# First stage of agent attention with an MLP: a ones column behind each value tile, 98-column key scores, and another order of the stage's work

## The chip, the cores and the metric

One core of a Trainium2 chip runs the kernel. The metric is device time in microseconds (us); the kernel before took 935.32 us, median of 3 runs.

## The reference

Two batches of 12480 queries, keys and values (128 channels) meet 49 agents. Then an MLP of 128 to 2048 to 128 channels with a PReLU runs over the 24960 rows.

```python
def sm(a, b):
    s = scale * (a @ b.transpose(0, 2, 1))
    s = s - s.max(-1, keepdims=True)
    e = np.exp(s)
    return e / (e.sum(-1, keepdims=True) + 1e-09)
a2k = sm(agents, k)
agent_v = a2k @ v
q2a = sm(q, agents)
attn = q2a @ agent_v
h = x @ w_in                       # x is attn, batch after batch
g = np.maximum(h, 0.0) + alpha * np.minimum(h, 0.0)
return g @ w_out
```

## The kernel before, in words

The main stage handles 52 chunks of 480 queries. `agent_v` is mixed into `w_in` ahead of it ("mix": `M_a`, `M_r`, and `L_a`, `L_b` for the linear part), so that a chunk is one product of its softmax `PT` with `M`, a ReLU split into `r_hi` and `r_lo`, and the second layer. The mixing needs `agent_v` of the batch. For batch 1 it is computed inside the first chunks of the main stage; for batch 0 it is computed in a stage of its own, the first stage, which takes the first 80 us or so. The change is there.

The first stage of before, each engine in the order in which its code is written (there is no scheduler; semaphores join them):

1. Keys. Tile 0 is a tail of two times 96 keys, then 12 pieces of 8 tiles of 128 keys. SyncE's queue (SP) loads a piece into a ring of 4 slots of `kv_s`; TensorE scores it against `agents` (L407), which holds the 98 agent columns of both batches and 30 columns of zeros, ScalarE saves the scores into `S` (L831), VectorE takes the maximum (L978). Between the pieces stand a maximum over the ReLU weights (L1141, L455, L459) and the scale and split of `w_out` (`weight_scale`, `weights_high` L860, `weights_low` L1087).
2. The maximum over all keys goes over TensorE to every partition (L446, L450) and into `k_shift`; GpSimd subtracts it from each piece (L381), ScalarE takes the exponential (L835).
3. TensorE turns the weights of the MLP (`turn_weights`, L431, 4 groups), scores the first two query chunks (L520), multiplies `w_in` by the linear `w_out` (`linear_weights`, L438), and multiplies each exponentiated piece with its values (`first_values`, L483: `S` is the stationary operand with 49 columns, the value tile streams through with 128 columns, even and odd tiles on two halves of the array). VectorE sums each piece (L1003) for the softmax denominators; `key_sums`, `key_sum` and `denominators` (L493) bring them to every partition, L1179 takes the reciprocal.
4. Handing over: `turn_values` (L489), `value_sums` (L497), `mix` (L501), `mix_rest`, `mix_linear`, the first `tiles` (L539) of the main stage, and then its first second layer (L556).

Queries of a chunk pass: scores on TensorE, `query_shift`, `query_exp`, `query_sum`, `query_norm`, then `query_hi` (ScalarE), `query_again` (GpSimd) and `query_lo` (VectorE, L1115) into `stack`. Once all three are there, SP's `turn(n, half)` issues four transposing DMAs `PT<-stack` (L275), waits until they have landed, and issues three copies `PR<-PT` (L279). SP is one queue in order: in the main stage it loads `q_s` for chunk n + 3 (L297) only after `turn(n + 1)`, and TensorE scores that chunk in the fourth second layer of chunk n:

```python
pe.wait_ge(in_q[1 - half], 16 * i + 32 + 16 * half)
...
second_layer(3, half, scores)
```

In chunk 0 this is `q_s[1]` with chunk 3, issued after `turn(1, 1)`, which waits for `query_lo(1)`.

Of the kernel before, what the change touches and what calls it, by code (L numbers as in the profile page):

```python
# [20 lines left out]
PIECE = 8 * KT  # L21
TAIL = (N - FULL * PIECE) // 2
# [19 lines left out]
def build(nc, kT, kTail, vP, vS, vTail, qT, agT, w_inT, w_out, alpha_col, out):  # L42
    ctx = ExitStack()
    with ctx:
# [9 lines left out]
        agents = sb("agents", [C, 128])  # L54
# [25 lines left out]
        kv_s = sb("kv_s", [128, 2 * RING, PIECE])  # L80
        k_tail = sb("k_tail", [C, B, 2 * TAIL])
        v_tail = sb("v_tail", [TAIL, B, 2 * C])
# [9 lines left out]
        av_rows = sb("av_rows", [128, C])  # L92
# [46 lines left out]
        def slot(p):  # L139
# [14 lines left out]
        consts, stack_zero, pool_step, dve_step = sem("consts"), sem("stack_zero"), sem("pool_step"), sem("dve_step")  # L154
# [10 lines left out]
        b_col, b_row, b_diag, b_top, b_shift, b_sum, b_den, b_dened, b_rows, b_turned, b_abs, b_vsum, b_vmax, b_av, b_avl = (  # L165
            sem(x) for x in ("b_col", "b_row", "b_diag", "b_top", "b_shift", "b_sum", "b_den", "b_dened", "b_rows",
# [55 lines left out]
        def value_tile(m, t):  # L222
            return kv_s[:, value_slot(m), t * C:(t + 1) * C]
# [4 lines left out]
        def _(sp):  # L228
            def load_keys(m):
                s = (m - 1) % RING  # L230
                if m > RING:

                    sp.wait_ge(k_scored, m - RING + 1)
                sp.dma_start(kv_s[:, s, :], kT[0, m - 1]).then_inc(in_k[s], 16)
# [15 lines left out]
            sp.dma_start(w_inT_s[:, :, :], w_inT).then_inc(in_wT, 16)  # L250
            for n in range(2):
                sp.dma_start(q_s[:, n, :], qT[n]).then_inc(in_q[n], 16)
            sp.dma_start(v_tail[:, 0, :], vTail[0]).then_inc(in_vt[0], 16)
            for m in range(1, FULL + 1):
                load_values(m)
# [25 lines left out]
            turn(0, 0)  # L281
# [3 lines left out]
            sp.dma_start(kv_s[:, 2, :], kT[1, 0]).then_inc(in_k[2], 16)  # L285
            for h in range(2):
                sp.dma_start(kv_s[:, h, :], kT[1, EARLY + h - 1]).then_inc(in_k[h], 16)
            sp.dma_start(v_tail[:, 1, :], vTail[1]).then_inc(in_vt[1], 16)
            turn(1, 1)

            def body(i, b, kind):
                for half in range(2):
# [30 lines left out]
        def _(pool):  # L323
            pool.memset(agents[:, B * A:128], 0.0).then_inc(consts, 1)
# [4 lines left out]
            pool.memset(rec_sel[:, :], 0.0).then_inc(consts, 1)  # L329
# [31 lines left out]
            pool.wait_ge(consts, 7)  # L361
# [42 lines left out]
        def _(pe):  # L404

            def wide_score(src, rows, bank, t):
                return pe.matmul(ps[0:rows, bank, t * 128:(t + 1) * 128], src, agents[:, :], start=True, stop=True)  # L407
# [61 lines left out]
            def first_values(m):  # L469
# [3 lines left out]
                else:  # L473
                    pe.wait_ge(in_v[(m - 1) % (2 * RING)], 16 * ((m - 1) // (2 * RING) + 1))
                pe.wait_ge(k_exped, m + 1)
                for t in range(count):
                    if m == 0:
                        rhs, rows = v_tail[:, 0, t * C:(t + 1) * C], TAIL
                    else:
                        rhs, rows = value_tile(m, t), KT  # L480

                    side = t % 2 * 64
                    mm = pe.matmul(ps[side:side + A, OUT, 0:C], S[0:rows, 0, at + t, :], rhs, start=(m == 0),  # L483
# [819 lines left out]
```

## Time and profile before

| | |
|---|---|
| median of 3 runs (lowest, highest) | 935.32 us (934.98, 936.42) |
| the profiled execution, its time and its span | 934.78 us, 933.1 us |
| TensorE (PE) busy | 98% of the span |
| VectorE, ScalarE, GpSimd busy | 68%, 55%, 12% |
| granted TensorE clock, mean | 0.992 |

The span runs from the first to the last instruction; the difference to the time lies around it. PE busy counts overlapping matmuls once, so 98% says that TensorE is seldom empty, not that it works at its peak. A float32 matmul stands in the profile as two instructions. The granted clock is 1.00 for 2.4 GHz and 0.50 for 1.2 GHz.

### The profile page before, as it was taken

To read this page: it belongs to the slowest core of one execution; us is meant where nothing else is said; L and a number is where in the kernel's file an instruction comes from. 1 tells how busy PE (TensorE), PEld (TensorE's weight loads), DVE (VectorE), ACT (ScalarE), POOL (GpSimd) and SP (SyncE) were. 2 spreads that over 40 slices of the span, in tenths; PEclk is the share of its full clock that TensorE was granted. 3 is DMA by queue.
4 is the path that set the end of the run, shared out by engine and by line. 5 is a ranking of instruction groups with operands and counts; after the bars stand their busy time and mean duration, and the time that the engine had idled before them with its cause. 6 is when DMAs were issued, how large, how long until landed. Compare 5 with 4: busy or idle time off the path is not lost.

```text
span 933.1 us, 16065 instructions
## 1 busy us (share of the span) xinstructions
PE 913.1 (98%) x5642; PEld 489.6 (52%) x5642; DVE 636.1 (68%) x927; ACT 514.6 (55%) x694; POOL 108.7 (12%) x140
## 2 busy tenths in 40 slices
PE   7899999999999999999999999999999999999998
PEld 6775555555545655654544444444444444444443
DVE  4567676676677777776776667676767676767664
ACT  2235555555556555555556555555555555555654
POOL 6310100100101001001001010101010101010101
PEclk9799999999999999999999999999999999999999
DMA  8751232222222322211111111111111111111110
GB/s 294 280 175 57 61 100 59 74 82 60 84 75 72 118 71 72 87 34 53 39 38 57 34 50 43 50 42 49 44 43 50 40 52 41 52 39 53 40 33 22
DMA packets 63206, 65.76 MB, mean 70 GB/s; under 512 B 38528, under 2 KB 57280, under 8 KB 62912
## 3 DMA queue, kind: packets, MB, share of 16 engines
q1 hardware_dynamic: 62880, 65.19, 22.9%
q8 instruction: 24, 0.39, 0.2%
q14 instruction: 14, 0.11, 0.0%
q10 hardware_dynamic: 288, 0.06, 0.0%
HBM read 40.49 MB, written 12.78 MB: 57 GB/s over the span
## 4 chain that ended last, share of the span: by engine, by line
PE 92%; DVE 2%; DMA 2%; issue 2%; SPq 1%; ACT 1%; POOLq 0%; POOL 0%
PE ps L556 54%; PE ps L539 17%; PE ps L546 7%; PE ps L520 3%; PE ps L566 2%; PE ps L718 2%; PE ps L407 2%; PE ps L712 1%; PE ps L483 1%; DMA kv_s<-kT 1%; PE ps L431 1%; PE ps L501 1%; DMA q_s<-qT 1%; SPq L275 0%; PE ps L438 0%
## 5 line engine op out<-in xcount | busy, mean ns | idle before, releaser
L1120 DVE SCALAR_TENSOR_TENSOR r_lo<-ps,r_hi 128x960 f16<-128x960 f32 x416 | 466.6, 1153 | 249.4 <-ACT r_hi L879 247.0
L879 ACT ACTIVATE r_hi<-ps 128x960 f16<-128x960 f32 x416 | 386.2, 967 | 175.4 <-PE ps L546 175.3
L556 PE MATMUL ps<-r_hi,w_hi 128*128 128x480 f16 x832 | 252.1, 369 | 1.9 <-DMA q_s<-qT 1.1
L556 PE MATMUL ps<-r_hi,w_lo 128*128 128x480 f16 x832 | 248.0, 366 | 0.0
L556 PE MATMUL ps<-r_lo,w_hi 128*128 128x480 f16 x832 | 240.7, 366 | 0.0
L539 PE MATMUL ps<-PT,M_a 128*128 128x480 f16 x832 | 203.3, 366 | 0.3 <-DVE r_lo L1120 0.2
L392 POOL TENSOR_TENSOR y<-y_relu,y_lin 128x480 f32<-128x480 f32 x52 | 62.4, 1200 | 616.6 <-ACT y_relu L958 444.3
L556 PEld LDWEIGHTS ps<-r_hi,w_lo 128*128 128x128 f16 x832 | 91.3, 110 | 68.8
L539 PEld LDWEIGHTS ps<-PT,M_a 128*128 128x128 f16 x832 | 81.1, 99 | 86.6 <-DVE r_lo L1120 2.6
L556 PEld LDWEIGHTS ps<-r_lo,w_hi 128*128 128x128 f16 x832 | 85.4, 106 | 71.2
L556 PEld LDWEIGHTS ps<-r_hi,w_hi 128*128 128x128 f16 x832 | 73.0, 106 | 85.3 <-issue 44.6
L941 ACT ACTIVATE y_lin<-ps,lin_unscale 128x480 f32<-128x480 f32 x52 | 34.4, 661 | 85.8 <-PE ps L566 85.8
L546 PE MATMUL ps<-PR,M_r 32*128 32x480 f16 x624 | 78.7, 372 | 0.0
L546 PE MATMUL ps<-PT,M_r 32*128 32x480 f16 x208 | 77.3, 371 | 0.0
L520 PEld LDWEIGHTS ps<-agents,q_s 128*120 128x120 f32 x416 | 70.3, 186 | 7.7 <-issue 0.4
L520 PE MATMUL ps<-agents,q_s 128*120 128x49 f32 x416 | 64.8, 242 | 0.0
L546 PEld LDWEIGHTS ps<-PT,M_r 32*128 32x128 f16 x208 | 18.8, 90 | 82.6 <-issue 82.2
L958 ACT ACTIVATE y_relu<-ps,out_unscale 128x480 f32<-128x480 f32 x52 | 34.4, 661 | 35.7 <-PE ps L556 35.7
L871 ACT ACTIVATE stack<-q_p 120x196 f16<-120x196 f32 x52 | 19.4, 373 | 62.1 <-DVE q_p L1111 62.1
L373 POOL TENSOR_TENSOR stack<-stack,ones 120x120 f16<-120x120 f16 x52 | 20.9, 402 | 181.1 <-ACT stack L871 181.1
L718 PEld LDWEIGHTS ps<-S,kv_s 128*128 128x128 f32 x192 | 33.1, 190 | 1.2
L712 PEld LDWEIGHTS ps<-agents,kv_s 128*128 128x128 f32 x176 | 30.9, 191 | 1.1
(143 smaller groups left out, 530.0 us busy)
## 6 DMA issues: line engine op xcount, KB each, us to landing
q_s<-qT SPq DMA_DIRECT2D x52, 240.0 KB, 2.7
out<-y SPq DMA_DIRECT2D x52, 240.0 KB, 2.0
kv_s<-kT SPq DMA_DIRECT2D x24, 512.0 KB, 4.1
kv_s<-vP SPq DMA_DIRECT2D x12, 512.0 KB, 7.6
kv_s<-vS SPq DMA_DIRECT2D x8, 768.0 KB, 4.3
PR<-PT SPq DMA_DIRECT2D x156, 32.0 KB, 1.9
PT<-stack SPq DMA_TRANSPOSE x208, 2.4
w_lin<-w_out SPq DMA_DIRECT2D x1, 1024.0 KB, 7.8
```

Source lines behind the costliest of these rows:

```text
L373: pool.tensor_tensor(stack[0:T, :, 2 * A:128], stack[0:T, :, REST:A], ones[0:T, 0:4 * SPARE].rearrange("p (t a) -> p t a", a=SPARE), ALU.m ...
L392: pool.tensor_tensor(y[:, half, :], y_relu[:, half, :], y_lin[:, half, :], ALU.add).then_inc(y_ready, 1)
L520: return pe.matmul(ps[0:T, SMALL, t * A:(t + 1) * A], q_s[:, half, t * T:(t + 1) * T], agents[:, b * A:(b + 1) * A], start=True, stop=True)
L539: pe.matmul(by_tile(ps[:, 2 * slot(p) + u, 0:CHUNK]), M_a[:, b, f:f + 128], tokens(PT, half), start=True, stop=False)
L546: mm = pe.matmul(by_tile(ps[:, 2 * slot(2 * q + u // 2) + u % 2, 0:CHUNK]), M_r[32 * u:32 * u + 32, b, q * 128:(q + 1) * 128], tokens(src[ ...
L556: mm = pe.matmul(ps[:, OUT, 0:CHUNK], w[:, 2 * p + u, :], r[:, s, u, :], start=(p == 0 and u == 0 and k == 0), stop=(p == PAIRS - 1 and u ...
L712: mm = pe.matmul(ps[:, SMALL, t * A:(t + 1) * A], kv_s[:, half, t * KT:(t + 1) * KT], agents[:, A:2 * A], start=True, stop=True)
L718: mm = pe.matmul(ps[:, SMALL, 0:A], second_s[:, at:at + C], S[:, 1, SECOND * n + (t + 2 - SECOND * FIRST_VALUES), :], start=(t == 0), stop ...
L879: act.activation(r_hi[:, p % RING, :, :], ps[:, at:at + 2, 0:CHUNK], ACT.Relu).then_inc(hi_ready, 1)
L941: act.activation(y_lin[:, half, :], ps[:, 2 * LIN_SLOT, 0:CHUNK], ACT.Copy, scale=lin_unscale[:, b, :]).then_inc(lin_saved, 1)
L958: act.activation(y_relu[:, half, :], ps[:, OUT, 0:CHUNK], ACT.Copy, scale=out_unscale[:, b, :]).then_inc(relu_saved, 1)
L1120: dve.scalar_tensor_tensor(out=r_lo[:, p % RING, :, :], in0=ps[:, at:at + 2, 0:CHUNK], scalar=0.0, in1=r_hi[:, p % RING, :, :], op0=ALU.ma ...
```

## The change

- Value tiles stand 129 columns apart in `kv_s` (`VC = C + 1`), each with a column of ones behind it, set by VectorE (`ones_of`). `first_values` streams 129 columns, so that column 128 of the product is the sum of the exponentials, the softmax denominator. A load of values is now written as 8 runs of 128 floats in each partition in place of one of 1024.
- For batch 0 `piece_sum`, `key_sums`, `key_sum` and `denominators` go. In their place: both halves of the denominator column scale the selection matrix (`den_sel`, one instruction each on VectorE and ScalarE), `denominators_spread` multiplies with ones (160 columns), VectorE adds EPS and takes the reciprocal over 128x160. Batch 1 keeps its sums.
- `agents` has 98 columns, without the zeros; wide scores stream 98 columns.
- TensorE: all of `turn_weights` stands around the exchange of the maxima, ahead of the values; `relu_max_row` moves from piece 7 to piece 10, `relu_max_everywhere` from piece 8 to after the turning; `linear_weights` moves ahead; the scores of chunk 2 (L520) move from behind the first `rest_of_quad` to between `value_sums` and the second half of the key tiles of batch 1.
- VectorE and ScalarE: `weight_scale`, `weights_high` and `weights_low` leave the key pieces and go behind the maxima; the shift of chunk 2 stands ahead of the first `mixed_low`, `query_lo(1)` behind the second, and the two key maxima of batch 1 behind `relu_lo(1, 1)`.
- SP: `w_lin` is loaded after the third key piece instead of the second, `w_inT` after the tenth, `q_s` of chunk 1 behind the first values, `turn(0, 0)` behind the first key load of batch 1.

```diff
-        agents = sb("agents", [C, 128])
+        agents = sb("agents", [C, B * A])
-        kv_s = sb("kv_s", [128, 2 * RING, PIECE])
+        kv_s = sb("kv_s", [128, 2 * RING, 8 * VC])
...
-                sp.dma_start(kv_s[:, value_slot(m), :], vP[m - 1]).then_inc(in_v[(m - 1) % (2 * RING)], 16)
+                sp.dma_start(values_in(m)[:, :, 0:C], vP[m - 1].rearrange("p (t c) -> p t c", c=C)).then_inc(in_v[(m - 1) % (2 * RING)], 16)
...
-                if m == 2:
+                if m == 3:
                     sp.dma_start(w_lin[:, :, :], w_out).then_inc(in_wo, 16)
+                if m == FULL - 2:
+                    sp.dma_start(w_inT_s[:, :, :], w_inT).then_inc(in_wT, 16)
...
-            turn(0, 0)
             sp.dma_start(k_tail[:, 1, :], kTail[1]).then_inc(in_kt[1], 16)
             sp.wait_ge(v_used, 2 * RING + 1)
-            sp.dma_start(kv_s[:, 2, :], kT[1, 0]).then_inc(in_k[2], 16)
+            sp.dma_start(kv_s[:, 2, 0:PIECE], kT[1, 0]).then_inc(in_k[2], 16)
+            turn(0, 0)
...
+            def denominators_spread():
+                pe.wait_ge(b_spread, 2)
+                pe.matmul(ps[:, K_BANK, 0:SEL], ones[:, :], den_sel[:, :], start=True, stop=True).then_inc(b_den, 1)
...
             act.wait_ge(v_used, FULL + 1)
-            act.activation(av_rows[64:64 + A, :], ps[64:64 + A, OUT, 0:C], ACT.Copy).then_inc(b_rows, 1)
+            act.activation(av_rows[64:64 + A, :], ps[64:64 + A, OUT, 0:VC], ACT.Copy).then_inc(b_rows, 1)
+            act.wait_ge(b_rows, 2)
+            act.activation(den_sel[64:64 + A, :], sel[64:64 + A, :], ACT.Copy,
+                           scale=av_rows[64:64 + A, C:VC]).then_inc(b_spread, 1)
...
+            dve.tensor_copy(av_rows[0:A, :], ps[0:A, OUT, 0:VC]).then_inc(b_rows, 1)
+            dve.wait_ge(b_rows, 2)
+            dve.tensor_scalar(den_sel[0:A, :], sel[0:A, :], av_rows[0:A, C:VC], None, ALU.mult).then_inc(b_spread, 1)
+            dve.wait_ge(b_den, 1)
+            dve.tensor_scalar(rec_sel[:, :], ps[:, K_BANK, 0:SEL], EPS, None, ALU.add).then_inc(b_dened, 1)
             dve.wait_ge(b_dened, 1)
-            then(dve.reciprocal(rec[:, :], den[:, :]))
+            then(dve.reciprocal(rec_sel[:, :], rec_sel[:, :]))
```

Where the order moves, first on TensorE (PE), from the first key piece to the first value tiles. Before:

```order
L407 MATMUL ps<-agents,kv_s 128x128 x56
L455 MATMUL ps<-ident,w_col 1x128
L407 MATMUL ps<-agents,kv_s 128x128 x8
L459 MATMUL ps<-relu_top,ones 128x1
L407 MATMUL ps<-agents,kv_s 128x128 x32
L446 MATMUL ps<-ident,k_col 49x128
L450 MATMUL ps<-k_diag,ones 128x49
L431 MATMUL ps<-turn_sign,w_inT_s 128x128 x4
L520 MATMUL ps<-agents,q_s 120x49 x4
L483 MATMUL ps<-v_tail,S 49x128 x2
```

TensorE of the change, the same place (L418 are the key scores, L442 the turned weights, L457 and L461 the exchange of the maxima, L449 the linear weights):

```order
L418 MATMUL ps<-agents,kv_s 128x98 x80
L466 MATMUL ps<-ident,w_col 1x128
L418 MATMUL ps<-agents,kv_s 128x98 x16
L442 MATMUL ps<-turn_sign,w_inT_s 128x128 x8
L457 MATMUL ps<-ident,k_col 49x128
L442 MATMUL ps<-turn_sign,w_inT_s 128x128 x4
L461 MATMUL ps<-k_diag,ones 128x49
L442 MATMUL ps<-turn_sign,w_inT_s 128x128 x4
L470 MATMUL ps<-relu_top,ones 128x1
L538 MATMUL ps<-agents,q_s 120x49 x4
L449 MATMUL ps<-w_lin,w_inT_s 128x128 x6
L496 MATMUL ps<-v_tail,S 49x129 x2
```

The two small matmuls leave the middle of the key pieces, and the weights' turning now fills the places of the two exchanges. Then VectorE (DVE) at the handing over, from the rest's low half to the second ReLU residue. Before (L1115 is `query_lo(1)`, L978 the two key maxima of batch 1, L1097 and L1099 the shift of chunk 2):

```order
L1077 TENSOR_TENSOR M_r<-ps,M_rh 128x512
L1115 TENSOR_TENSOR stack<-q_p,stack 120x4x49
L1081 SCALAR_TENSOR_TENSOR L_a<-L_a,gate,ps 32x128
L1083 TENSOR_TENSOR L_b<-ps,L_rh 32x128
L978 TENSOR_REDUCE k_top<-S 128x49 x2
L1120 SCALAR_TENSOR_TENSOR r_lo<-ps,r_hi 128x960
L1072 SCALAR_TENSOR_TENSOR M_a<-M_a,gate,ps 32x512
L1097 TENSOR_REDUCE q_top<-ps 120x4
L1099 TENSOR_TENSOR q_e<-ps,q_top 120x196
L1072 SCALAR_TENSOR_TENSOR M_a<-M_a,gate,ps 32x512 x2
```

VectorE of the change, the same place (`query_lo(1)` is L1137 here):

```order
L1099 TENSOR_TENSOR M_r<-ps,M_rh 128x512
L1103 SCALAR_TENSOR_TENSOR L_a<-L_a,gate,ps 32x128
L1105 TENSOR_TENSOR L_b<-ps,L_rh 32x128
L1142 SCALAR_TENSOR_TENSOR r_lo<-ps,r_hi 128x960
L1094 SCALAR_TENSOR_TENSOR M_a<-M_a,gate,ps 32x512
L1137 TENSOR_TENSOR stack<-q_p,stack 120x4x49
L1094 SCALAR_TENSOR_TENSOR M_a<-M_a,gate,ps 32x512 x2
L1142 SCALAR_TENSOR_TENSOR r_lo<-ps,r_hi 128x960
L1000 TENSOR_REDUCE k_top<-S 128x49 x2
```

`query_lo(1)` now stands behind the first ReLU residue and the second `mixed_low`, the key maxima behind the second residue, and the shift of chunk 2 is gone from here.

## Rows read from the trace of the kernel before

**Rows 1.** The page: busy time by engine, and two DMA issues.

```profile
PE 913.1 (98%) x5642; PEld 489.6 (52%) x5642; DVE 636.1 (68%) x927; ACT 514.6 (55%) x694; POOL 108.7 (12%) x140
...
q_s<-qT SPq DMA_DIRECT2D x52, 240.0 KB, 2.7
...
w_lin<-w_out SPq DMA_DIRECT2D x1, 1024.0 KB, 7.8
```

**Rows 2.** PE's timeline, key pieces: start, us, engine and line, idle before.

```profile
11.27 9.20 PE L407 MATMUL ps<-agents,kv_s 128*128 128x128 f32 x80 [1.28 <-DMA kv_s<-kT]
22.41 0.38 PE L455 MATMUL ps<-ident,w_col 128*1 128x128 f32 x2 [1.95 <-DVE w_col L1141]
...
25.01 7.41 PE L407 MATMUL ps<-agents,kv_s 128*128 128x128 f32 x64
35.91 0.66 PE L446 MATMUL ps<-ident,k_col 128*49 128x128 f32 x2 [3.48 <-DVE k_col L987]
```

**Rows 3.** Busy time by stretch; PEclk is the granted clock.

```profile
20.00:22.40 2.40, 0.47 (x5) 0.29 (x4) 2.40 (x3) 0.50 (x1) 0.00 (x0) 1.00 0.88 283
...
34.90:45.10 10.20, 8.54 (x44) 7.36 (x46) 5.32 (x10) 2.69 (x6) 6.89 (x9) 0.50 0.75 298
...
65.60:69.00 3.40, 3.40 (x24) 2.82 (x23) 1.34 (x6) 0.89 (x3) 0.40 (x1) 0.50 0.95 311
```

**Rows 4.** PE's timeline, weights, queries and values.

```profile
37.81 2.07 PE L431 MATMUL ps<-turn_sign,w_inT_s 128*128 128x128 f32 x8
...
45.50 1.16 PE L431 MATMUL ps<-turn_sign,w_inT_s 128*128 128x128 f32 x8
...
49.70 1.04 PE L520 MATMUL ps<-agents,q_s 128*120 128x49 f32 x8
50.57 1.57 PE L438 MATMUL ps<-w_lin,w_inT_s 128*128 128x128 f32 x12
...
60.23 2.83 PE L483 MATMUL ps<-kv_s,S 128*49 128x128 f32 x48
65.35 0.39 PE L493 MATMUL ps<-k_col,ones 128*128 128x49 f32 x2 [2.29 <-DVE k_col L1013]
65.67 1.95 PE L483 MATMUL ps<-kv_s,S 128*49 128x128 f32 x16
```

**Rows 5.** GpSimd's and VectorE's timelines: the shifts, two reciprocals.

```profile
38.21 11.42 POOL L381 TENSOR_TENSOR S<-S,k_shift 128x98 f32<-128x98 f32 x13 [20.04 <-DVE k_shift L996]
...
61.01 0.18 DVE L1107 RECIPROCAL q_rec<-q_den 120x4 f32<-120x4 f32 x1
...
66.03 0.47 DVE L1179 RECIPROCAL rec<-den 128x49 f32<-128x49 f32 x1
```

**Rows 6.** PE's timeline, the handing over.

```profile
71.47 1.12 PE L501 MATMUL ps<-w_in_s,av_m 128*128 128x512 f32 x2
...
75.36 1.04 PE L520 MATMUL ps<-agents,q_s 128*120 128x49 f32 x8
76.23 2.81 PE L501 MATMUL ps<-w_in_s,av_m 128*128 128x512 f32 x6
79.79 0.36 PE L556 MATMUL ps<-r_hi,w_hi 128*128 128x480 f16 x1 [0.75 <-DVE q_e L1099]
```

**Rows 7.** VectorE, SP's queue, and PE's first query score in chunk 0.

```profile
74.91 0.35 DVE L1115 TENSOR_TENSOR stack<-q_p,stack 120x196 f16<-120x196 f32 x1
...
77.99 0.76 DVE L1072 SCALAR_TENSOR_TENSOR M_a<-M_a,gate,ps 32x512 f16<-32x512 f16 x1
...
75.35 4.93 SPq L275 DMA_TRANSPOSE PT<-stack  x4
82.76 1.79 SPq L279 DMA_DIRECT2D PR<-PT  x3
84.59 0.58 SPq L297 DMA_DIRECT2D q_s<-qT  x1
...
87.85 0.31 PE L520 MATMUL ps<-agents,q_s 128*120 128x49 f32 x2
```

More of the change, by code:

```diff
@@ L247, in _ @@
                 load_keys(m)
-                if m == 2:
+                if m == 3:
                     sp.dma_start(w_lin[:, :, :], w_out).then_inc(in_wo, 16)
[L250 to L254, printed above, removed]
+                if m == FULL - 2:
+                    sp.dma_start(w_inT_s[:, :, :], w_inT).then_inc(in_wT, 16)
+            sp.dma_start(q_s[:, 0, :], qT[0]).then_inc(in_q[0], 16)
+            load_tail(0)
+            load_values(1)
+            sp.dma_start(q_s[:, 1, :], qT[1]).then_inc(in_q[1], 16)
+            for m in range(2, FULL + 1):
                 load_values(m)
@@ L300, in body @@
                         sp.wait_ge(k_scored, n + (FULL + EARLY + 2))
-                        sp.dma_start(kv_s[:, half, :], kT[1, n + (EARLY + 1)]).then_inc(in_k[half], 16)
+                        sp.dma_start(kv_s[:, half, 0:PIECE], kT[1, n + (EARLY + 1)]).then_inc(in_k[half], 16)
                     if kind == TOP:
@@ L406, in wide_score @@
             def wide_score(src, rows, bank, t):
-                return pe.matmul(ps[0:rows, bank, t * 128:(t + 1) * 128], src, agents[:, :], start=True, stop=True)
+                return pe.matmul(ps[0:rows, bank, t * 128:t * 128 + B * A], src, agents[:, :], start=True, stop=True)
             def tail_scores(b, bank):
@@ L477, in first_values @@
                     if m == 0:
-                        rhs, rows = v_tail[:, 0, t * C:(t + 1) * C], TAIL
+                        rhs, rows = v_tail[:, 0, t, :], TAIL
                     else:
-                        rhs, rows = value_tile(m, t), KT
+                        rhs, rows = values_in(m)[:, t, :], KT
                     side = t % 2 * 64
-                    mm = pe.matmul(ps[side:side + A, OUT, 0:C], S[0:rows, 0, at + t, :], rhs, start=(m == 0),
+                    mm = pe.matmul(ps[side:side + A, OUT, 0:VC], S[0:rows, 0, at + t, :], rhs, start=(m == 0),
                                    stop=(m == FULL and t >= 6), skip_group_check=True)
@@ L601, in _ @@
             query_scores(1)
[L603 to L606 removed]
             first_values(5)
[L608 removed]
             first_values(6)
+            weight_max_rows()
             first_values(7)
[L611 removed]
             first_values(8)
@@ L616, in _ @@
             first_values(11)
-            pe.wait_ge(b_shift, 1)
-            denominators(0, K_BANK)
             first_values(12)
@@ L698, in body @@
                     if kind == SUMS and half == 1:
-                        denominators(1, SMALL)
+                        denominators(SMALL)
                     if kind == MIX:
@@ L1186, in _ @@
-            dve.tensor_copy(av_rows[0:A, :], ps[0:A, OUT, 0:C]).then_inc(b_rows, 1)
+            query_sum(0)
+            query_norm(0)
+            query_lo(0)
+            dve.wait_ge(lin_w_ready, 1)
+            dve.tensor_reduce(w_col[:, 2:3], lin_w[:, :], AX.X, ALU.max, apply_absolute_value=True).then_inc(wmax_col, 1)
+            query_shift(1)
+            weight_max_top()
+            weight_max_save()
+            weights_low()
+            query_sum(1)
+            query_norm(1)
+            dve.wait_ge(v_used, FULL + 1)
@@ L1190, in _ @@
             values_scaled(0, K_BANK)
+            query_shift(2)
             mixed_low(0, 0, F_BANK[0])
             rest_low(0, REST_BANK[0])
+            linear_low(0)
+            relu_lo(0, 0)
+            mixed_low(0, 1, F_BANK[1])
             query_lo(1)
-            linear_low(0)
+            mixed_low(0, 2, F_BANK[2])
+            mixed_low(0, 3, F_BANK[3])
+            relu_lo(1, 1)
             for m in range(EARLY):
```

160 lines of the change are left out of this document (68 added, 92 removed).

## The prediction

> **What bounds the kernel now.** I read the page first: PE is busy for 98% of the span, all other engines far less [rows 1], so time is won only where PE waits, works at the lower clock, or has work taken away. The timeline of PE puts nearly all its idle time ahead of 80 us: 1.28 us for a key load, 1.95 us for the maximum over the ReLU weights (L1141), 3.48 us for the key maximum [rows 2], 2.29 us for the sums of the exponentials (L1013) [rows 4], 0.75 us for the shift of a query chunk [rows 6]. The stretches then show the clock: it was 0.50 of 2.4 GHz, that is 1.2 GHz, for 10.2 us from 34.9 us on, behind and inside the 3.48 us wait, and for 3.4 us from 65.6 us on, behind the 2.29 us wait; the 1.95 us wait did not bring it down [rows 3]. What the low level costs is seen in one shape: 8 L431 take 2.07 us in it and 1.16 us at full clock [rows 4].
>
> I follow one marker, the start of the first second layer of the main stage (L556), at 79.79 us [rows 6]. Behind it all stages are the same in both kernels, save one load that the last term takes up.
>
> **98 columns: nothing.** A key piece is 16 instructions; 64 of them take 7.41 us, less some 0.25 us in which the last drains, so 0.112 us each and 1.79 us a piece [rows 2]. The query scores stream only 49 columns past 120 stationary ones and still start every 0.109 us (8 from 49.70 to 50.57 us) [rows 4]. The stationary side sets the pace, so I take 0 for 30 columns fewer. The bounds are 0 and 30/128 of 0.112 us, 0.026 us for each of 192 instructions, 5.0 us. The Trainium skill, page "TensorE: Matmul & The Clock Gate", section "LDWEIGHTS (loading the stationary operand)", says the same as my choice: a load takes as long as the stationary operand has columns. The values stream 129 for 128, under 1%, below 0.1 us.
>
> **Keys: 2.8 us earlier.** Before, the third piece waits until 11.27 us, behind the 1 MB of `w_lin` [rows 2]; that lands 7.8 us after its issue, at about 10 us [rows 1]. Now `w_lin` is one piece later, so the third piece is scored at once and the fourth waits for the same bytes, until about 12.5 us. Four pieces are then scored at 14.4 instead of 14.9 us: 0.5 us. The 1.95 us wait goes, because the small matmul stands three pieces later and the reduction (2.3 us) ends under pieces 8 and 9. One small matmul with its change of operands (0.3 us) leaves the pieces for a later place. The keys end at 29.6 instead of 32.4 us. `w_inT` (1 MB, some 2.5 us of transfer) is pushed between pieces 10 and 11; pieces were landing about a microsecond ahead of their use there, so I take 0 and keep up to 1.5 us for the range.
>
> **Exchange of the maxima: the clock stays up.** After the last save VectorE needs only one piece and two small instructions, since `w_lo` (2.3 us) is gone from there: the column maximum is there 2.0 us after the last score, at 31.6 us, against 3.5 us before (35.9 less 32.4) [rows 2]. PE turns two weight groups meanwhile (2 times 0.95 us) and is idle for well under 1 us. That is below the 1.95 us after which the clock stayed up, so I count everything from here to 53 us at full clock.
>
> **PE from 31.6 us to the last value.** At full clock, from [rows 4] with 0.1 us for each change between operand kinds: two small matmuls for the maxima, two for the weights and one for the ReLU maximum, 5 times 0.3 us; two weight groups 2.0; two query chunks 1.9; `linear_weights` 32 instructions at 0.112, with its changes 4.1; the tail's values 0.45; twelve value pieces at 0.88 us (48 instructions in 2.83 us are three, less draining) 10.5, changes 0.7. Sum 21.2 us, so 52.8 us; with two short waits I take 53.0. Before, the same point is 67.6 (65.67 plus 1.95) [rows 4]. So 14.6 us are won, and the 3.48, 2.29 and the low clock are what they are made of. Two engines must keep up. GpSimd's 13 shifts take 11.42 us once the shift is known [rows 5], at 33.9 instead of 38.2 us, so they end at 45.3. ScalarE follows with the exponentials but has 2.0 us of `w_hi` between them; its last is done at 48.5, and PE wants it at 52. Both hidden, with 3 us to spare.
>
> **From the last value to the mix: 1.8 us longer.** Before it is 67.6 to 71.5, 3.9 us, [rows 4, 6], since the denominators were ready. Now they hang on the last value: copy 0.3, scaling the selection 0.3, the 160-column product 0.5, adding EPS 0.35, a reciprocal over 160 columns. 4 columns take 0.18 us and 49 take 0.47 [rows 5], so 6.4 ns a column and 1.2 us for 160. Then the product 0.35, the absolute value 0.25, `value_sums` 0.25: 3.5 us. PE adds the queries of chunk 2 (0.97 us, which stood later before) and half a key piece (0.9): 5.7 us. The mix begins at 58.7 instead of 71.5.
>
> **From the mix to the second layer: 1.35 us shorter.** Before 8.3 us [rows 6]. The 0.97 us of queries is gone, and so is the 0.75 us wait for the shift; instead `mixed_low` (0.76 us, ended at 78.75 before [rows 7]) and the three mixes (2.81 us) end about together, 3.0 us after `rest_of_quad`. 6.9 us, so the marker is at 65.6: 14.2 us earlier.
>
> **A new wait in chunk 0: 3.9 us given back.** `query_lo(1)` ended at 75.26, and SP's `turn(1, 1)` began 0.1 us later. Four transposing DMAs, a wait for them and three copies put the load of chunk 3's queries at 84.59, 9.2 us after the turn began [rows 7], landing 2.7 us (median) later [rows 1]. PE scores it from 87.85 on, one 0.2 us matmul into the fourth second layer [rows 7]: 7.85 us after the marker, and the load came in just in time. Before, `query_lo(1)` ends 4.5 us ahead of the marker. Now it stands behind the residue and the second `mixed_low`, which itself releases the marker, so it ends 0.35 us behind it. The load lands 0.35 + 0.1 + 8.2 to 9.2 + 2.7 = 11.4 to 12.4 us after the marker (8.2 where the last transpose lands as fast as the three ahead of it), PE wants it at 7.85. That is 3.5 to 4.5 us; I take 3.9. Queued behind the load on SP are a key load and `turn(2)`; the turn also waits for chunk 0's last quad, which is late by the same amount, so they cost nothing more. PE has nothing in its queue to do meanwhile.
>
> **The clock after that wait.** 3.9 us is more than either wait that brought the clock down. After 2.29 us it was at 0.50 for 3.4 us: half of that is lost, 1.7 us. A part may fall into the idle time itself. I take 1.2, from 0 to 3.5. The same could follow the waits at 53 to 57 us (some 1.7 us in pieces), which I leave to the range.
>
> **The sum.** -14.2 + 3.9 + 1.2 = -9.1 us, against the 934.78 us of the profiled execution: 925.7. The runs' median is 0.54 us above it, so 926.2.
>
> **Rivals.**
> 1. *The queries are there in time* (0.08). For it: each half chunk of the main stage hides such a load. Against it: those turns start from their own chunk's `query_lo`, long ahead. Without wait and clock loss 921.1 us.
> 2. *Fewer streamed columns do shorten the key scores* (0.05). A stream of 98 for 128 columns would save up to 0.026 us for each of 192 instructions, and the loads would take about half of it back: 2.5 us, 923.7 us. Against it is the pace of the 49-column scores [rows 4]. The Trainium skill, page "TensorE: Matmul & The Clock Gate", section "Back-to-back issue gap", lets the spacing go with the streamed columns; by that rule this rival would be right, and the trace speaks against it in this shape.
> 3. *More waits in the first stage* (0.19). `w_inT` holds up pieces 11 and 12, the ring pushes the maxima out, and the clock falls there or in the hand-over: each of these 1.5 to 3.5 us. 929 to 932 us; I put 0.03 of it within 0.2% of before.
> 4. *The value loads hold up the values, slower than before* (0.05). A load is 8 runs in each partition now. SP takes about 0.6 us to issue a load or copy with one run [rows 7]. If issuing went with the runs it would be 4.6 us. The first value load stands at about 23 us, the twelfth must be issued by 48, so up to 2.1 us each is hidden. From 2.9 us each on, the twelfth is 9 us late and the gain is gone; at 4.6 us it would be some 956 us. For it: no row shows such a load. Against it: the size makes no difference to the issue, and a transposing DMA, of 128 rows of 256 bytes, takes 1.2 us [rows 7], which would be hidden.
>
> My forecast itself has 0.63.
>
> **How the numbers follow.** The likeliest case gives 926.2, by its own terms 923.8 to 929.5 (wait 3.5 to 4.5, clock 0 to 3.5, the first stage 1.5 either way). The range takes in rivals 1 and 2 nearly whole and the near part of rival 3: 921.5 to 930.5. A measurement of this kernel tells about 0.2%, 1.9 us, from no change. Faster by more 0.92, within 0.03, slower 0.05.
>
> **What would show it.** In the profile after: L418 instructions still 0.112 us apart; no wait over 1 us between 13 and 53 us and PEclk 1.00 there; a reciprocal of about 1.2 us; L574's first start near 65.6 us; and a wait of PE for the DMA `q_s<-qT` of 3.5 to 4.5 us, 7.85 us after it, perhaps with a low clock behind it. I am wrong if that wait is missing, if PE waits for `kv_s<-vP`, or if the clock falls ahead of 53 us.

## The result, and the profile after

The changed kernel takes 931.28 us (median of 15 runs, 928.23 to 936.13) against 935.39 us for the kernel before on the same chip (933.19 to 937.20): a ratio of 0.9954, 95% interval 0.9940 to 0.9967. It is faster, by 4.1 us where 9.1 were forecast, and lies 0.8 us above the range. The profiled execution took 929.73 us, 5.05 less than the one before; forecast was 925.7.

The page of the changed kernel: busy time by engine (as in [rows 1]), and the packets of all transfers. Before there were 63,206, of them 57,280 under 2 KB: the 12 value loads in runs of 512 bytes make the difference.

```profile
PE 911.3 (98%) x5642; PEld 488.6 (53%) x5642; DVE 627.2 (68%) x914; ACT 515.1 (56%) x695; POOL 108.4 (12%) x138
...
DMA packets 74149, 65.75 MB, mean 71 GB/s; under 512 B 38528, under 2 KB 69760, under 8 KB 73856
```

TensorE's timeline of the changed kernel answers to [rows 2, 4, 6, 7]; columns are start, us, line, count, and the idle time ahead with what ended it. The marker of the prediction is L574 here, L556 before.

```profile
4.91 20.25 PE L418 MATMUL ps<-agents,kv_s 128*128 128x98 f32 x160 [0.68 <-DMA kv_s<-kT]
25.08 0.38 PE L466 MATMUL ps<-ident,w_col 128*1 128x128 f32 x2
28.03 5.44 PE L418 MATMUL ps<-agents,kv_s 128*128 128x98 f32 x32 [2.57 <-DMA kv_s<-kT]
33.31 1.98 PE L442 MATMUL ps<-turn_sign,w_inT_s 128*128 128x128 f32 x16
35.21 0.42 PE L457 MATMUL ps<-ident,k_col 128*49 128x128 f32 x2
...
52.95 3.74 PE L496 MATMUL ps<-kv_s,S 128*49 128x129 f32 x64
56.62 0.58 PE L418 MATMUL ps<-agents,k_tail 128*96 128x98 f32 x4
...
60.42 0.39 PE L515 MATMUL ps<-av_abs,ones 128*128 128x49 f32 x2 [1.43 <-DVE av_abs L1063]
...
62.43 1.05 PE L519 MATMUL ps<-w_in_s,av_m 128*128 128x512 f32 x2
...
69.42 0.36 PE L574 MATMUL ps<-r_hi,w_hi 128*128 128x480 f16 x1 [0.33 <-DVE M_a L1094]
...
80.84 0.56 PE L574 MATMUL ps<-r_hi,w_hi 128*128 128x480 f16 x1 [3.51 <-DMA q_s<-qT]
81.19 0.49 PE L538 MATMUL ps<-agents,q_s 128*120 128x49 f32 x2
```

Stretches of the changed kernel: the two at the low clock, and the shifts and values between them. Columns are the stretch and its length, the busy us (with the count of instructions) of PE, PEld, DVE, ACT and POOL, then the granted clock, the DMA share and GB/s.

```profile
29.30:32.70 3.40, 3.40 (x18) 3.40 (x18) 1.46 (x4) 0.50 (x1) 0.00 (x0) 0.50 1.16 306
36.00:52.00 16.00, 16.00 (x193) 14.30 (x192) 7.98 (x20) 9.70 (x20) 11.90 (x14) 1.00 1.06 278
80.50:87.30 6.80, 6.46 (x24) 3.53 (x24) 1.44 (x3) 0.66 (x1) 0.00 (x0) 0.50 0.14 54
```

VectorE's timeline of the changed kernel, with the denominators' reciprocal and `query_lo(1)`.

```profile
58.52 1.15 DVE L1200 RECIPROCAL rec_sel<-rec_sel 128x160 f32<-128x160 f32 x1
...
69.34 0.36 DVE L1137 TENSOR_TENSOR stack<-q_p,stack 120x196 f16<-120x196 f32 x1
```

SP's queue in the changed kernel, behind it: `turn(1, 1)` and the load of chunk 3's queries.

```profile
69.80 5.17 SPq L288 DMA_TRANSPOSE PT<-stack  x4
76.12 1.86 SPq L292 DMA_DIRECT2D PR<-PT  x3
78.02 0.58 SPq L310 DMA_DIRECT2D q_s<-qT  x1
```

Two places differ from the plan. Key piece 11 waits 2.57 us for its load, whose 512 KB are queued behind the 1 MB of `w_inT`, and the granted clock falls to 0.50 behind that wait, for 3.4 us. And the foreseen `q_s` wait, 3.51 us, is followed by 6.8 us at 0.50. All between 33.31 and 57.96 us went as planned: no wait, clock 1.00.

A ledger of the profiled executions. The marker moved from 79.79 [rows 6] to 69.42 us: -10.37. From it to chunk 3's first query score it was 8.06 us before [rows 6, 7] and is 11.77 now: +3.71. From there to chunk 4's first query score it was 17.09 us and is 19.83 us: +2.74. At the full clock this stretch takes 16.88 us (e2, e3, e11) or 17.09 (before, e4), so the low clock costs 2.7 to 3.0. Behind that, TensorE waited 0.42 and 0.71 us for `q_s` at 529 and 546 us before, 0.17 us in all now: -0.96. The remaining -0.17 is not placed. The sum is -5.05.

### The profile page after: what moved, and what is told of

It reads as the page before. It is cut to its first block, busy times and chain, and to the rows that moved or that the text cites. A ratio compares the mean times of both kernels' runs of the same rounds, so it can differ in the third digit from the quotient of the medians.

```text
span 928.0 us, 16051 instructions
## 1 busy us (share of the span) xinstructions
PE 911.3 (98%) x5642; PEld 488.6 (53%) x5642; DVE 627.2 (68%) x914; ACT 515.1 (56%) x695; POOL 108.4 (12%) x138
## 3 DMA queue, kind: packets, MB, share of 16 engines
q1 hardware_dynamic: 73824, 65.19, 23.3%
## 4 chain that ended last, share of the span: by engine, by line
PE 93%; DMA 3%; SPq 2%; issue 2%; DVE 0%; POOLq 0%; ACT 0%
PE ps L574 55%; PE ps L557 18%; PE ps L564 7%; PE ps L538 3%; PE ps L584 2%; DMA kv_s<-kT 2%; PE ps L736 2%; PE ps L418 2%; PE ps L730 1%; PE ps L496 1%; SPq L288 1%; DMA q_s<-qT 1%; DMA PT<-stack 1%; PE ps L519 1%; PE ps L449 0%
## 5 line engine op out<-in xcount | busy, mean ns | idle before, releaser
L574 PE MATMUL ps<-r_hi,w_hi 128*128 128x480 f16 x832 | 252.4, 369 | 4.0 <-DMA q_s<-qT 3.7
L574 PE MATMUL ps<-r_hi,w_lo 128*128 128x480 f16 x832 | 248.4, 367 | 0.0
L574 PE MATMUL ps<-r_lo,w_hi 128*128 128x480 f16 x832 | 241.1, 367 | 0.0
L574 PEld LDWEIGHTS ps<-r_hi,w_lo 128*128 128x128 f16 x832 | 91.4, 111 | 68.8
L574 PEld LDWEIGHTS ps<-r_lo,w_hi 128*128 128x128 f16 x832 | 85.6, 106 | 71.2
L574 PEld LDWEIGHTS ps<-r_hi,w_hi 128*128 128x128 f16 x832 | 73.0, 106 | 87.5 <-issue 43.4
L889 ACT ACTIVATE stack<-q_p 120x196 f16<-120x196 f32 x52 | 19.4, 373 | 67.1 <-DVE q_p L1133 64.5
L1000 DVE TENSOR_REDUCE k_top<-S 128x49 f32<-128x392 f32 (+2 forms) x26 | 20.0, 777 | 18.0 <-ACT S L849 18.0
```

The source lines that it names most:

```text
L574: mm = pe.matmul(ps[:, OUT, 0:CHUNK], w[:, 2 * p + u, :], r[:, s, u, :], start=(p == 0 and u == 0 and k == 0), stop=(p == PAIRS - 1 and u ...
L1000: dve.tensor_reduce(k_top[:, b, m, :], by_agent(piece(b, m)), AX.X, ALU.max).then_inc(k_maxed, 1)
```

## Experiments

Each gives the median and the ratio to the kernel before, which ran beside it on the same chip. For reading them: from the fastest to the slowest execution it is 2.3 to 5.6 us in each experiment and 7.9 us in the 15 of the changed kernel, and this goes largely with their mean granted clock. Of the four of e3_both, two with 1.000 took 922.6 and 923.9 us, those with 0.997 and 0.996 took 924.3 and 925.8. So a profile's time is not its kernel's median, and the waits are compared in the profiles. These scatter too: the wait for the first key piece, which no edit touches, is 0.4 to 2.3 us long in the sixteen profiles.

**e1_winT_last.** The 1 MB behind all keys.

```
-                if m == FULL - 2:
+                if m == FULL:
                     sp.dma_start(w_inT_s[:, :, :], w_inT)...
```

> The changed kernel with one edit: w_inT is loaded behind the twelfth key piece instead of behind the tenth. Theory A (1 MB stands ahead of piece 11 in one queue while the keys are already scored as fast as they land): the 2.57 us wait of PE for kv_s<-kT and the 3.4 us at half clock behind it go, keys are scored by 29.6 us instead of 33.4, w_inT lands just as the turning wants it (wait below 0.5 us), and the time falls by about 4 us, 927.3 us. Rival B (the value loads, 8 short runs in each partition, hold up the key pieces): the order of w_inT changes little, 931 us, and the wait before piece 11 stays. Rival C (what counts is all bytes until the weights are turned): the wait moves to the first L442, with the same length, 930 to 931 us.

932.69 us, 0.9963 (0.9948 to 0.9977): no gain. TensorE's timeline of e1_winT_last:

```profile
31.51 2.05 PE L442 MATMUL ps<-turn_sign,w_inT_s 128*128 128x128 f32 x16 [0.68 <-DMA w_inT_s<-w_inT]
...
53.43 1.09 PE L496 MATMUL ps<-kv_s,S 128*49 128x129 f32 x16 [0.23 <-DMA kv_s<-vP]
55.04 1.09 PE L496 MATMUL ps<-kv_s,S 128*49 128x129 f32 x16 [0.52 <-DMA kv_s<-vP]
...
58.84 1.70 PE L418 MATMUL ps<-agents,kv_s 128*128 128x98 f32 x8 [1.27 <-DMA kv_s<-kT]
```

The wait for key piece 11 is gone and the turning starts 1.8 us sooner, although the first key piece came 1.26 us later than in the changed kernel's profile. But the values and the next batch's first keys then come late, and the clock is at 0.50 from 59.2 to 66.1 us. The marker is at 72.0 and the `q_s` wait behind it 4.03 us.

**e2_lo_early.** `query_lo(1)` back where the kernel before had it.

```
             rest_low(0, REST_BANK[0])
+            query_lo(1)
             linear_low(0)
             relu_lo(0, 0)
             mixed_low(0, 1, F_BANK[1])
-            query_lo(1)
```

> The changed kernel with one edit: query_lo(1) on VectorE back behind rest_low, ahead of linear_low, as in the kernel before. Theory A: SP's turn(1, 1) begins some 3.5 us earlier, the load of q_s[1] lands in time for the fourth second layer of chunk 0, the 3.51 us wait and the 6.8 us at half clock behind it go: 3.5 + 3.1, about 6.5 us less, 924.8 us. Rival D (the clock is down at this place in any case, since it had to fall once after the exchange): only the wait goes, 927.8 us. Rival E (the turn moves, but the DMA is late anyway): 931 us.

926.25 us, 0.9890 (0.9872 to 0.9907): 5.0 us below the changed kernel. TensorE's timeline of e2_lo_early, at the place of the `q_s` wait:

```profile
79.44 0.36 PE L574 MATMUL ps<-r_hi,w_hi 128*128 128x480 f16 x1 [0.48 <-issue]
```

Of the 3.51 us wait 0.48 us are left. The profile names no releaser for them, but the load lands just then, at 79.35 us. The clock stays at 1.00 from 34.7 us on; before that it was at 0.50 for 6.8 us, from within the wait for key piece 11 (1.98 us here).

**e3_both.** e1 and e2 together.

> The changed kernel with both edits, w_inT behind piece 12 and query_lo(1) behind rest_low. Theory A: the two losses are independent and add: 4 + 6.5 us less, 920.8 us, marker (first second layer) near 65.6 us and no wait over 1.5 us ahead of chunk 1. Rival: with the keys 4 us earlier another wait comes up, most likely for the last value piece (its load lands at 53.4 us now and would be wanted at 52) or for q_s: 923 to 925 us.

924.09 us, 0.9871 (0.9855 to 0.9887). With the `q_s` wait nearly out of the way (0.50 us left), e1's edit brings 2.2 us over e2 and not the 4 expected, and the two intervals overlap. The profile still has waits of 0.30 us for values and 1.26 us for the next keys, and the low clock from 57.8 us on for 6.8 us.

**e4_load_first.** `query_lo(1)` stays late, but SP issues the load first.

```
             load_tail(1)
+            sp.wait_ge(q_scored, 2)
+            sp.dma_start(q_s[:, 1, :], qT[3]).then_inc(in_q[1], 16)
             turn(1, 1)
```

> The changed kernel with query_lo(1) left where it is, but on SP the load of chunk 3's queries issued ahead of turn(1, 1) instead of behind it. Theory A (the wait is a place in SP's queue and nothing else): the same as the run with query_lo(1) early, 924.8 us. Rival F (the late turn is itself what costs): PE waits later, for PT of chunk 1 (L557) some 14 us behind the marker, and the time is above 927 us.

924.96 us, 0.9877 (0.9859 to 0.9896). SP's queue in e4_load_first:

```profile
66.15 0.59 SPq L303 DMA_DIRECT2D q_s<-qT  x1
73.71 5.12 SPq L288 DMA_TRANSPOSE PT<-stack  x4
```

The turn begins 0.38 us behind the marker, as in the changed kernel, and TensorE has no `q_s` wait. The median is 6.3 us below the changed kernel. So it was the load's place in SP's queue, not VectorE's lateness as such.

**e5_values_whole.** On e3_both, value pieces load as one run. This kernel leaves the column of ones out of the value pieces: the 129th column is the next tile's first value, so batch 0's denominators are wrong numbers. It shows times alone.

```
-    sp.dma_start(values_in(m)[:, :, 0:C], vP[m - 1].rearrange("p (t c) -> p t c", c=C))
+    sp.dma_start(kv_s[:, value_slot(m), 0:PIECE], vP[m - 1])
...
-    rhs, rows = values_in(m)[:, t, :], KT
+    rhs, rows = kv_s[:, value_slot(m), t * C:t * C + VC], KT
```

> The kernel of e3_both (924.1 us) with each value piece loaded as one run of 4,096 bytes per partition instead of eight runs of 512 bytes into places 516 bytes apart; the matmuls still read 129 columns per value tile, but the 129th is now the next tile's first value, so the softmax sums of the first batch are wrong numbers and the output differs from the reference. Theory (the short runs are what limits the value loads): value loads land one per 1.3 us instead of 1.75, the next batch's first key load lands before 54 us instead of at 57.5, the waits of 0.30 us for values and 1.27 us for that load go, the granted clock does not fall at 58 us, and the time is about 921 us (920 to 922). Rival (the loads are limited by something that the two layouts share): spacing stays at 1.7 us and the time at 924 us.

924.59 us, 0.9890 (0.9873 to 0.9906), a miss in time: no gain over e3_both. Its profiled execution took 920.01 us, has no wait for values or for the next keys, and has the marker at 66.16. Four further executions took 922.6 to 925.6 us with mean clocks of 0.997 to 0.995: the clock fell somewhere in them that no profile shows.

**e6_128_columns.** On e3_both, zero columns back behind the agents.

```
-        agents = sb("agents", [C, B * A])
+        agents = sb("agents", [C, 128])
...
-  pe.matmul(ps[0:rows, bank, t * 128:t * 128 + B * A], src, agents[:, :], ...)
+  pe.matmul(ps[0:rows, bank, t * 128:(t + 1) * 128], src, agents[:, :], ...)
```

> The kernel of e3_both (924.1 us) with 30 zero columns back behind the agents, so each key tile streams 128 columns and not 98. Forecast's term (98 columns save nothing, key tiles are paced at 0.112 us by something else): spacing stays 0.112 us and the time at 924.1, within 0.5. Rival (a streamed column costs its 0.42 ns at full clock): 112 tiles by 12.5 ns are 1.4 us more, 925.5 us.

923.06 us, 0.9878 (0.9862 to 0.9894). TensorE's timeline of e6_128_columns:

```profile
4.89 19.99 PE L419 MATMUL ps<-agents,kv_s 128*128 128x128 f32 x160 [0.40 <-DMA kv_s<-kT]
```

160 instructions of 128 columns take as long as 160 of 98 (19.98 us in e5_values_whole, 20.25 in the changed kernel); 32 of them at the full clock take 3.84 us here and 3.81 in e9_after_whole. The term of 0 holds.

**e7_key_load_sooner.** On e3_both.

```
-            sp.wait_ge(v_used, 2 * RING + 1)
+            sp.wait_ge(v_used, 2 * RING)
             sp.dma_start(kv_s[:, 2, 0:PIECE], kT[1, 0]).then_inc(in_k[2], 16)
```

> The kernel of e3_both (924.1 us) with the next batch's first key load released by the eighth finished value piece (which is the last reader of its buffer) and not by the ninth, about 1 us sooner. Theory (that load is late because of where it is issued): it lands 0.5 to 1 us sooner than 57.5 us, the wait of 1.27 us for it shrinks as much, and the time is 923 us, down to 922 if the clock no longer falls there. Rival (the load only queues behind the value loads, which keep all 16 DMA engines busy): it lands when it did, 924.1 us.

924.10 us, 0.9891 (0.9876 to 0.9907). The load was issued at 50.4 us (50.6 in e3_both), landed at 57.3 (57.5), and its wait is again 1.27 us: the rival. SP was busy with the loads ahead of it until 50.4, and the transfer then queues behind the value loads.

**e8_sums_on_vector.** e3_both's order with VectorE's sums of before, values 128 wide and no ones.

```
-VC = C + 1
+VC = C
...
+                dve.wait_ge(k_exped, m + 1)
+                piece_sum(0, piece(0, m), m)     # m = 0 .. 12, other rows between
...
+            denominators(0, K_BANK)              # between value pieces 11 and 12
```

> The order of e3_both (924.1 us) without the column of ones: VectorE sums each exponential piece as in the kernel before, TensorE adds the sums over the partitions between value pieces 11 and 12, values lie 128 wide and load as one run of 4,096 bytes. Theory (the ones column frees VectorE, which is not what sets the end here, and costs the short runs): value waits and the wait for the next batch's keys go as in e5_values_whole, and the hand-over from the last value to the mix is the 3.9 us of the kernel before and not 5.8: 919 to 921 us. Rival (VectorE's 13 sums of about 0.45 us push the rows of queries and the shifts late, or the sums end after the last value piece): 924 us or more.

927.78 us, 0.9931 (0.9915 to 0.9947): 3.7 us slower than e3_both, the rival. TensorE's timeline of e8_sums_on_vector:

```profile
59.11 0.64 PE L505 MATMUL ps<-k_col,ones 128*128 128x49 f32 x2 [5.26 <-DVE k_col L1027]
```

VectorE's timeline of the same kernel:

```profile
51.25 2.33 DVE L1101 SCALAR_TENSOR_TENSOR w_lo<-w_relu,w_scale,w_hi 128x2048 f16<-128x2048 f32 x1
53.51 1.51 DVE L1017 TENSOR_REDUCE k_top<-S 128x49 f32<-128x392 f32 x2
...
57.91 0.81 DVE L1017 TENSOR_REDUCE k_top<-S 128x49 f32<-128x392 f32 x1
58.75 0.21 DVE L1027 TENSOR_TENSOR k_col<-k_col,k_top 128x49 f32<-128x49 f32 x1
```

With the new order VectorE has no room for 13 sums of 0.8 us (the expectation had put 0.45 each): it has no gap from 47 to 59 us and makes TensorE wait 5.26 us, with the clock at 0.50 for 6.8 us from within that wait. The column of ones pays here, short runs and a longer hand-over included, at least with the sums in this order.

**e9_after_whole.** The edit of e5_values_whole on the changed kernel alone, again without the ones.

> The changed kernel (931.3 us) with nothing else altered than the layout of e5_values_whole: each value piece loads as one run of 4,096 bytes per partition, and the 129th column of each value tile is its neighbour's first value, so the first batch's softmax sums are wrong numbers. Theory (short runs slow the value loads, but with w_inT ahead of key piece 11 the stage is late for that piece anyhow): loads land 1.3 us apart, the waits for key piece 11 and for q_s stay, and the time is 930 to 931 us, a gain under 1.5. Rival (the short runs alone cost what the forecast missed): 927 us.

928.80 us, 0.9948 (0.9928 to 0.9968): 2.5 us below the changed kernel, between theory and rival, and the two intervals overlap. The stretch from 30 to 38 us, when value loads are under way and, in its first 3 us, what is left of query and weight loads, in three profiles, with the DMA share and GB/s as the last two numbers. The kernel before:

```profile
30.00:38.00 8.00, 3.87 (x27) 3.16 (x26) 6.39 (x9) 1.00 (x2) 0.00 (x0) 0.81 1.03 388
```

The changed kernel:

```profile
30.00:38.00 8.00, 8.00 (x56) 7.49 (x54) 4.06 (x10) 2.37 (x5) 0.60 (x2) 0.83 1.15 294
```

e9_after_whole:

```profile
30.00:38.00 8.00, 7.69 (x63) 7.01 (x62) 4.83 (x16) 4.14 (x9) 3.10 (x5) 1.00 1.03 407
```

The layout of the loads is what slows the transfer: 294 GB/s for 407, with all engines busy in both. From the second value piece to the eighth one lands every 1.82 us in the changed kernel, every 1.32 here. Key piece 11 waits 0.89 us here, behind the same 1 MB.

**e10_winT_last_whole.** e1's edit and e5's on the changed kernel, again without the ones.

> e1_winT_last (932.7 us) with the value layout of e5_values_whole, so sums of the first batch are again wrong numbers. Theory (moving w_inT behind the keys gained nothing only because value loads in short runs then came late): the waits for key piece 11, for values and for the next batch's first key load are all gone, the q_s wait of about 4 us stays, the mix starts near 60 us, and the time is 927 to 928 us, 4 to 5 below e1_winT_last and below e9_after_whole by 3. Rival (the two are independent): as far below e1_winT_last as e9_after_whole is below the changed kernel.

928.08 us, 0.9931 (0.9914 to 0.9948): 4.6 us below e1_winT_last, as the theory had it, but only 0.7 below e9_after_whole where it said 3. TensorE's timeline of e10_winT_last_whole has two waits for loads between 6 and 80 us:

```profile
30.36 2.05 PE L442 MATMUL ps<-turn_sign,w_inT_s 128*128 128x128 f32 x16 [1.04 <-DMA w_inT_s<-w_inT]
...
78.14 0.56 PE L574 MATMUL ps<-r_hi,w_hi 128*128 128x480 f16 x1 [3.69 <-DMA q_s<-qT]
```

No value or key load is waited for. So what took e1's gain back was the slower value loads.

**e11_winT_quarters.** On e2_lo_early.

```
-                if m == FULL - 2:
-                    sp.dma_start(w_inT_s[:, :, :], w_inT).then_inc(in_wT, 16)
+                if m in (6, 7, 8, 9):
+                    f = m - 6
+                    sp.dma_start(w_inT_s[:, 4 * f:4 * f + 4, :], w_inT[:, 4 * f:4 * f + 4, :])...
```

> The kernel of e2_lo_early (926.3 us) with w_inT loaded in four quarters of 256 KB, one behind each of the key loads 6 to 9, instead of whole behind key load 10. Theory (what made key piece 11 late is one transfer of 1 MB ahead of it, while each key piece leaves about 0.5 us of the DMA engines over): key waits stay under 0.7 us each, the turning of the weights starts near 29.6 us with no wait for w_inT, then the value loads limit as in e3_both, and the time is 922 to 923 us. Rival (the DMA engines have nothing left over between key loads either): some key piece waits 1.5 us or more and the time is 926 us.

922.73 us, 0.9880 (0.9860 to 0.9899), as the theory expected. TensorE's timeline of e11_winT_quarters:

```profile
23.48 3.98 PE L419 MATMUL ps<-agents,kv_s 128*128 128x98 f32 x32 [0.77 <-DMA kv_s<-kT]
...
31.35 1.98 PE L443 MATMUL ps<-turn_sign,w_inT_s 128*128 128x128 f32 x16
```

The longest key wait behind the fourth piece is 0.77 us, the clock is 1.00 from 10 us to the end of the main stage, the marker is at 67.8. But the turning begins at 31.35 us and not near 29.6 as expected. The first value load lands at 31.15 us, 2.4 sooner than in e3_both, and nothing waits for values or for the next keys.

**e12_places_576_apart.** On e11_winT_quarters, only the pitch of the value tiles.

```
+VP = 144
-    return kv_s[:, value_slot(m), :].rearrange("p (t c) -> p t c", c=VC)
+    return kv_s[:, value_slot(m), :].rearrange("p (t c) -> p t c", c=VP)
```

> The kernel of e11_winT_quarters (922.7 us) with the value tiles 576 bytes apart in a partition instead of 516: eight runs of 512 bytes as before, but each begins at a multiple of 64 bytes, and the sums column is right behind each tile still. Theory (what slows the value loads is that a run is short): loads land one per 1.75 us as in e11, 922.7 us. Rival (what slows them is where a run begins): they land one per 1.3 us as in e9_after_whole, and the time is 921 us.

924.25 us, 0.9877 (0.9859 to 0.9894). The same stretch of e12_places_576_apart:

```profile
30.00:38.00 8.00, 7.72 (x63) 7.04 (x63) 4.81 (x14) 3.60 (x9) 2.43 (x4) 1.00 1.03 300
```

300 GB/s where e11 has 289 and whole runs 407, but this stretch has other loads in it too, and places 516 bytes apart give anything from 279 to 305 in it. The landings tell more. From the second value piece to the eighth one lands every 1.58 us here. With places 516 bytes apart it is every 1.73 to 1.88 us in ten profiles, with whole runs every 1.27 to 1.33 in five. So the answer of this one profile lies between theory and rival: a third to a half of the loss goes with where the runs begin, the rest with their length. The time can't tell, since nothing waits for values in e11 either.

**e13_after_again.** The changed kernel, unaltered.

> The changed kernel once more, for a second profile. Theory (key piece 11 is late by chance of how fast w_inT goes through, between 0.9 and 2.6 us): its wait is anywhere in that range, the q_s wait is again 3.5 to 4.2 us, 931 us. Rival (the short value runs behind it hold it up each time): the wait is again 2 us or more.

932.11 us, 0.9962 (0.9948 to 0.9976). Key piece 11 waits 1.82 us, `q_s` 4.16. With 2.57 (after), 1.98 (e2) and 1.57 (e4) that is four profiles between 1.6 and 2.6 with short runs behind the 1 MB, against the one of 0.89 with whole runs. The scatter of about 1 us is shown; whether the short runs take part in it is not settled.

**e14_after_quarters.** e11's edit on the changed kernel alone.

> The changed kernel (931.3 us) with w_inT in four quarters behind key loads 6 to 9 and nothing else. Theory (the forecast's step that took 0 for w_inT is what failed at the keys, and nothing later makes up for it): no wait of over 0.8 us at the keys, mix near 61 us, first second layer near 67.8 us, q_s wait 3.5 to 4.2 us with the clock falling behind it, and the time is 928 us. Rival (as in e1_winT_last, something later takes it back): 931 us.

929.42 us, 0.9940 (0.9926 to 0.9953), between theory and rival: 1.9 us below the changed kernel and 2.7 below e13, which ran beside it. TensorE's timeline of e14_after_quarters:

```profile
58.78 0.39 PE L516 MATMUL ps<-av_abs,ones 128*128 128x49 f32 x2 [1.44 <-DVE av_abs L1064]
...
60.78 1.79 PE L520 MATMUL ps<-w_in_s,av_m 128*128 128x512 f32 x2
...
69.36 0.36 PE L575 MATMUL ps<-r_hi,w_hi 128*128 128x480 f16 x1 [0.33 <-DVE M_a L1095]
```

The turning begins at 31.30 us, 2.0 sooner than in the changed kernel, and the mix 1.65 us sooner, but in this execution the clock fell there (61.0 to 64.4 us), behind the 1.44 us wait for the denominators' chain: the two `mix` instructions take 1.79 us for 1.05. So the marker is where it was. The load of `q_s` is again what chunk 0 waits for: 3.59 us, until 80.86, with the landing at 80.77.

## Why the prediction was wrong

The sign and most of the steps held; the size fell short by 5 us at the median, 4.0 in the profiles. Step by step:

- **98 columns, 0:** right. Spacing stayed 0.112 us, and e6 gives the columns back at no cost. The Trainium skill, page "TensorE: Matmul & The Clock Gate", section "LDWEIGHTS (loading the stationary operand)", agrees in that the stationary columns count. Its section "Back-to-back issue gap" lets the spacing of a single matmul go with the streamed columns and has both operations set it in a stream of loads and matmuls; for 98 against 128 columns in this 32-bit shape no share of the streamed side is seen.
- **Keys 2.8 us earlier:** this is the step that failed, in its last sentence. `w_inT` was given "some 2.5 us of transfer", pieces were "landing about a microsecond ahead of their use there", and the forecast went on "so I take 0". Its own two numbers leave a wait of 1.5 us. A lead of one microsecond gives no reason for 0, and the 1.5 us went into the range alone. The wait measured 2.57 us, and 1.57 to 1.98 us in the three other profiles with the same loads (e4, e13, e2); with whole value runs it was 0.89 (e9). The clock at 0.50 for 3.4 us in the scores behind it cost another 1.6 us (5.44 us for 32 instructions, 3.81 in e9). Up to piece 10 the keys were some 0.6 us ahead of the plan, so the turning began at 33.3 us and not at 29.6. The marker's whole delay of 3.8 us is there already at that point. What exceeds 1.5 us is how fast the 1.5 MB of `w_inT` and piece 11 came in behind piece 10: in 5.2 us here (landings at 22.8 and 27.99 us), some 300 GB/s, with query and value loads under way beside them; in 5.1, 4.2 and 3.9 us in e2, e13 and e4, and in 3.8 in e9. Why it varies stays open. Taking this wait away gains 1.9 us by itself (e14) and 3.5 with the `q_s` wait nearly gone (e11 against e2), both with intervals that overlap. No place tried for the 1 MB gave the planned 29.6: the turning began at 31.1 to 31.4 us with quarters, and at 30.0 to 31.5 us with it behind all keys.
- **Exchange, values, shifts:** right. Turning to last value took 23.3 us, forecast 23.4; the clock was at 1.00 throughout; the exponentials were hidden.
- **Hand-over 5.7 us:** right, 5.8 (56.62 to 62.43), with the reciprocal at 1.15 us against 1.2. The parts that the forecast lists for it add up to 5.4, though (3.5, 0.97 and 0.9), and 5.7 went into the sum; the chain put at 3.5 us took 4.0. **Mix to marker 6.9:** 7.0.
- **The new `q_s` wait, 3.9 us:** right, in its chain too: 3.51 here, 3.6 to 4.2 in the others. e4 removes it by one edit and e2 all but 0.48 us of it, and e4 shows that its seat is SP's queue.
- **The clock after that wait, 1.2 us:** mis-sized. It measured 2.7 to 3.0 us (6.8 us at half clock, less the idle time in it). The forecast took the 3.4 us behind a 2.29 us wait as its pattern; behind 3.5 to 4.2 us it was 6.8 us in five of six profiles. The whole `q_s` step with its clock was put at 5.1 us and is worth 5.0 by e2, 6.3 by e4, 6.7 by e14 against e11, 8.6 by e1 against e3.
- **Behind chunk 4:** 1.1 us came back that the forecast did not have, 0.96 of it in two waits for `q_s` at 529 and 546 us that are smaller now. That the shifted times made them so is not shown.

With the measured values, -14.2 + 3.8 + 3.7 + 2.7 - 1.1 = -5.1. The median lies 1.5 us above the profiled execution. Only five of the other fourteen runs have a lower mean clock than its 0.994, so the clock alone does not explain this, and no trace shows where the others lose.

Rival 3 came true in place, mechanism and size (929 to 932 us), beside the forecast's own `q_s` wait. Rival 4 looked for the cost of short runs in SP's issue. That did grow, from 0.43 to 0.92 us at the median of the twelve value loads and to 2.9 at most, far from the 4.6 of rival 4, and the DMA engines were busy all along. What slows the loads is in the transfer, which rival 4 didn't price. In the changed kernel it makes no wait that the profile shows, but it is next in line: mending `w_inT` alone by moving it back (e1) runs into it, mending both (e10) does not. How much of it the changed kernel itself pays stays open: e9's 2.5 us are within the intervals.

e3_both with its variants e6 and e7, and e11_winT_quarters with e12, at 923 to 924 us, are the best that compute the reference, 7 to 8.5 us under the changed kernel and not to be told apart.

## What to carry to other kernels

When a large load is slipped in front of a small one that is just in time, charge it with its transfer time less the lead that the small one has, and not with 0; allow for a slower rate beside other loads, and charge the clock behind the wait as well. When work on a vector engine is moved back, follow the DMA queue that waits for it to the loads behind: reordering one load (e4) was worth as much as moving the work (e2). Padding a tile for an extra column can be right and still turn one long run into many short ones; look at packets and GB/s after it, not only at the issue times.

## What was not expected of the hardware

- **Short runs at full occupation.** Value loads in 512-byte runs, 516 bytes apart, moved 279 to 305 GB/s from 30 to 38 us in ten profiles, with a DMA share of 1.05 to 1.17, loads in 4,096-byte runs 388 to 407 GB/s with 1.03. The Trainium skill, page "DMA: Bandwidth & Descriptors", section "Specifications", sets the least transfer for line rate at 512 bytes; here loads in runs of that size lose about a quarter of the rate, and the measurement decides. Placing the runs at multiples of 64 bytes took the landings from one in 1.73 to 1.88 us to one in 1.58 (e12), whole runs to one in 1.3.
- **The clock does not go by the wait alone.** Behind waits of 1.26 to 1.44 us at 57 to 63 us it fell in some executions (e3, e1: 6.8 us; e4, e12, e14: 3.4 us) and not behind others of the same length (e6, e7, the changed kernel). It fell behind 1.57 us at the keys in e4, too. Before, 1.95 us left it up and 2.29 us brought it down [rows 2, 3, 4]. From chunk 3's scores to chunk 4's the same work took 16.9 to 17.1 us at full clock, 18.5 with 3.4 us at 0.50, and 19.4 to 19.8 with 6.8 us.
